# Second slot of a mixture-of-experts kernel: order of loads, index, low terms and register reads

## The chip, the cores and the metric

One Trainium2 chip, one of its cores. The metric is the device time of one execution in microseconds (us), median of three runs. TensorE (matmuls and 128x128 transposes), VectorE, ScalarE and GpSimd work at the same time and are ordered by semaphores alone; SyncE (SP) issues most of the DMAs. GpSimd issues the indirect ones (gather and scatter of rows).

## The reference

```python
def _attn_ref(x, state):                 # x (8, 8, 512, 64), state (8, 8, 32, 64)
    xread = softmax(scale * x @ state.T) @ state
    sread = softmax(scale * state @ x.T) @ x
    return concatenate([xread, sread], axis=2)
# heads are put side by side: 4352 rows of 512
def _moe_ref(x, expert_emb, tau, w1, w2):     # 8 experts, w1 512x1024, w2 1024x512
    logits = normalised(x) @ normalised(expert_emb).T / tau
    e = argmax(logits); gate = softmax(logits)[e]
    return gate * (maximum(x @ w1[e], 0) @ w2[e])
def _moe2_ref(x, w_in, w_out, alpha):         # 512 -> 2048 -> 512
    h = x @ w_in
    return (maximum(h, 0) + alpha * minimum(h, 0)) @ w_out
```

Everything is float32. Each row goes through the two matrices of the one expert with the highest logit.

## The kernel before, in words

Products of float32 are made of three faster ones: each operand is split into a rounded high term and a low term (what rounding left), and `three` (L391 to L395) adds high x high, high x low and low x high. ScalarE mostly makes the high term of a tile, VectorE the low one by a subtraction.

The kernel has three stages. **Attention** runs over the 8 batches (`turn`); its rows go to DRAM (`rows_x`). **Routing and experts** (about 131 to 628 us of the profile): VectorE finds each row's expert and its place, and TensorE turns this into lists of rows (`gather_idx`, `scatter_idx`), 128 rows of one expert to a slot. A slot is: GpSimd gathers the 128 rows into `xg`; TensorE turns them (`transpose_x`, L1621 on), ScalarE and VectorE split them (`xgT_hi`, `xgT_lo`); TensorE makes the hidden rows in two halves (`hidden`, 24 products of 512 columns), VectorE copies each half to `hid`, TensorE turns it, ScalarE and VectorE split it with the relu (`hidT_hi`, `hidT_lo`); TensorE makes the result (`result`, 24 products), ScalarE copies it to `yrow`, GpSimd scatters it. The **last stage** (from about 640 us) is the second network, and the diff does not touch it.

Slots 0 and 1 are written out by hand, because slot 0 starts before the lists are complete: its rows come from a short list of expert 0 (`first_...`), and its work is interleaved with the making of the full lists. VectorE's order there is: `place` (where each row goes in its slot), the small `table` (for each expert its first slot, the number of slots that convert weights, and its end), the two `hidT_lo` of slot 0, the index lists, the low terms of weight chunk 3, the norms and the gate, `xgT_lo` of slot 1. TensorE's is: 8 warm-up products, the rank counts (L1652), `transpose_x(0)`, `hidden`, the index products (L1666), `result` of slot 0, `transpose_x(1)`. GpSimd issues the second gather (L715) as soon as `gather_idx` is complete, with `scatter_idx` and the table to be waited for afterwards (`index_ready` up to `INDEXED`, 8).

The weights of an expert are 4 chunks of 1 MB. SP loads each into one of 4 places of `stage`, ScalarE rounds it to `w_hi`, VectorE subtracts it to `w_lo` (`rest_chunk`, L1001 on). Chunks 0 to 3 (expert 0) pass during attention and slot 0; chunks 4 to 7 (expert 1) are loaded from L499 on, each after the one before has landed, and 6 and 7 only after the second gather has. Chunk 4 needs place 0 (chunk 2 is converted), chunk 5 needs place 1 (chunk 3 is converted).

After that all engines loop over pairs of experts. At the start of each expert ScalarE and VectorE read four numbers of the table into registers (`slots_of`, L386 to L389): start, turns, mid (= start + turns) and end. For expert 0 the start is 1; for each other it is the end of the one before. In the first `turns` slots (at most 2) they also convert the next expert's chunks; an expert with fewer slots has the rest converted at its end. For the first four experts VectorE also makes four sums of blocks of the last stage's weights.

## Time and profile before

| | |
|---|---|
| median of 3 runs | 1375.01 us (1374.06 to 1376.0) |
| the profiled execution's own time | 1372.04 us |
| its span in the profile | 1370.1 us |
| mean granted TensorE clock | 0.992 |
| busy: TensorE, VectorE, ScalarE, GpSimd | 98%, 62%, 31%, 12% of the span |
| experts end at | 321, 371, 383, 440, 503, 565, 615 and 628 us |

The profile is of one execution. Its times are counted from the start of the span; the chain that ended last is 90% TensorE. "Idle before" is what an engine had no work for ahead of an instruction, with the instruction that released it. TensorE's clock is given as a share of 2.4 GHz: 1.00 or, at its lower level, 0.50 (1.2 GHz); a number between them is a mean over a stretch. The end of a matmul is modelled, so the starts are what to go by. A few matmul records are missing.

### The profile page before, as it was taken

How to read it: one execution, taken by the hardware profiler on the slowest of the kernel's cores; microseconds unless marked ns; L12 is line 12 of the kernel's file. 1: busy time of each engine (PE TensorE's matmuls, PEld its weight loads, DVE VectorE, ACT ScalarE, POOL GpSimd, SP SyncE). 2: the span in 40 equal slices, each digit the busy share in tenths (PEclk: the TensorE clock that was granted, in tenths of full speed). 3: DMA queues.
4: the chain of work that ended last, by engine and by line, in shares of the span. 5: the costliest groups of instructions: out<-in, count | busy, mean ns of one | idle time of the engine just before them, and what ended most of it. 6: DMA issues, size and time to landing. Idle time of an engine off the chain costs nothing.

```text
span 1370.1 us, 22457 instructions
## 1 busy us (share of the span) xinstructions
PE 1337.0 (98%) x7820; PEld 1152.7 (84%) x7821; DVE 842.8 (62%) x1106; ACT 424.6 (31%) x611; POOL 166.6 (12%) x228
## 2 busy tenths in 40 slices
PE   8999799999989999998999999999999999999998
PEld 7888578888868888887999999999978888888887
DVE  7898652225474534438667776678966666666652
ACT  6887341114242322325112121113222222222221
POOL 3563121112121121211000000000000000000000
PEclk9999899999999999999999999999999999999999
DMA  8884361114466416234444324343444444444463
GB/s 277 286 280 156 134 221 45 38 46 160 139 225 219 161 44 254 83 124 162 155 141 137 132 109 143 132 144 132 145 126 115 115 115 115 115 115 115 119 118 54
DMA packets 180258, 193.41 MB, mean 141 GB/s; under 512 B 24832, under 2 KB 130304, under 8 KB 179712
## 3 DMA queue, kind: packets, MB, share of 16 engines
q1 hardware_dynamic: 172960, 172.41, 40.4%
q0 software_dynamic: 6112, 19.93, 4.2%
q10 hardware_dynamic: 1152, 0.66, 0.2%
q8 instruction: 17, 0.28, 0.1%
q14 instruction: 17, 0.14, 0.0%
HBM read 125.07 MB, written 67.37 MB: 140 GB/s over the span
## 4 chain that ended last, share of the span: by engine, by line
PE 90%; DVE 6%; DMA 2%; issue 1%; ACT 1%; DVEq 0%; POOL 0%; SPq 0%; ACTq 0%; POOLq 0%
PE ps_p L393 13%; PE ps_p L395 13%; PE ps_p L394 13%; PE ps_y L393 5%; PE ps_y L395 5%; PE ps_y L394 5%; PE ps_h L393 5%; PE ps_h L395 5%; PE ps_h L394 5%; PE ps_o L394 5%; PE ps_o L393 5%; PE ps_o L395 5%; PE ps_hT L1630 2%; PE ps_xT L1624 1%; DVE a L1066 1%; PE ps_sr L1514 1%
## 5 line engine op out<-in xcount | busy, mean ns | idle before, releaser
L393 PE MATMUL ps_p<-b_hi,w_hi 128*128 128x272 f32 x896 | 258.9, 289 | 4.1 <-DVE b_lo L1348 4.1
L395 PE MATMUL ps_p<-b_hi,w_lo 128*128 128x272 f32 x896 | 259.1, 289 | 0.0
L394 PE MATMUL ps_p<-b_lo,w_hi 128*128 128x272 f32 x896 | 259.1, 289 | 0.0
L393 PEld LDWEIGHTS ps_p<-b_hi,w_hi 128*128 128x128 f32 x896 | 169.1, 189 | 5.1 <-DVE b_lo L1348 5.1
L395 PEld LDWEIGHTS ps_p<-b_hi,w_lo 128*128 128x128 f32 x896 | 169.4, 189 | 0.0
L394 PEld LDWEIGHTS ps_p<-b_lo,w_hi 128*128 128x128 f32 x896 | 168.7, 188 | 0.0
L1287 DVE COPY hid<-ps_h 128x512 f32<-128x512 f32 x72 | 49.8, 691 | 171.5 <-PE ps_h L395 166.3
L393 PE MATMUL ps_h<-w_hi,xgT_hi 128*128 128x512 f32 x296 | 121.6, 411 | 3.1 <-DVE xgT_lo L1159 3.1
L393 PE MATMUL ps_y<-w_hi,hidT_hi 128*128 128x512 f32 x296 | 123.3, 417 | 1.2 <-DVE w_lo L1004 0.8
L1415 DVE SCALAR_TENSOR_TENSOR neg<-gt,alpha 128x2048 f32<-128x2048 f32 x33 | 75.6, 2292 | 71.5 <-DMA gt<-acts 71.5
L1426 DVE TENSOR_TENSOR g_lo<-gt,g_hi 128x2048 fp32r<-128x2048 f32 x34 | 77.9, 2292 | 65.5 <-ACT g_hi L964 65.5
L395 PE MATMUL ps_h<-w_hi,xgT_lo 128*128 128x512 f32 x296 | 117.6, 397 | 0.0
L394 PE MATMUL ps_h<-w_lo,xgT_hi 128*128 128x512 f32 x296 | 117.4, 396 | 0.0
L395 PE MATMUL ps_y<-w_hi,hidT_lo 128*128 128x512 f32 x296 | 116.5, 394 | 0.0
L394 PE MATMUL ps_y<-w_lo,hidT_hi 128*128 128x512 f32 x296 | 116.3, 393 | 0.0
L393 PE MATMUL ps_p<-w_hi,g_hi 128*128 128x512 f32 x272 | 107.5, 395 | 1.3 <-issue 1.3
L395 PE MATMUL ps_o<-w_hi,g_lo 128*128 128x512 f32 x272 | 107.4, 395 | 0.0
L394 PE MATMUL ps_o<-w_lo,g_hi 128*128 128x512 f32 x272 | 107.4, 395 | 0.0
L393 PE MATMUL ps_o<-w_hi,g_hi 128*128 128x512 f32 x272 | 107.4, 395 | 0.0
L394 PE MATMUL ps_p<-w_lo,g_hi 128*128 128x512 f32 x272 | 107.4, 395 | 0.0
L395 PE MATMUL ps_p<-w_hi,g_lo 128*128 128x512 f32 x272 | 107.4, 395 | 0.0
L1163 DVE SCALAR_TENSOR_TENSOR hidT_lo<-ps_hT,hidT_hi 128x512 fp32r<-128x512 f32 x74 | 51.1, 691 | 87.9 <-ACT hidT_hi L860 87.9
(258 smaller groups left out, 2345.6 us busy)
## 6 DMA issues: line engine op xcount, KB each, us to landing
acts<-gb SPq DMA_DIRECT2D x128, 272.0 KB, 2.1
stage<-in_moe_w SPq DMA_DIRECT2D x32, 1024.0 KB
gt<-acts SPq DMA_DIRECT2D x32, 1024.0 KB, 6.1
xN_all<-in_xN SPq DMA_DIRECT2D x8, 1024.0 KB, 6.3
rows_x<-xrow SPq DMA_DIRECT2D x32, 256.0 KB, 2.7
out_rows<-orow SPq DMA_DIRECT2D x32, 256.0 KB, 2.0
yz<-rows_y SPq DMA_DIRECT2D x30, 256.0 KB
xs_all<-in_xT SPq DMA_DIRECT2D x7, 1024.0 KB, 6.8
```

The source lines that it names most:

```text
L393: pe.matmul(out, s_hi, m_hi, start=start, stop=False)
L394: pe.matmul(out, s_hi, m_lo, start=False, stop=False)
L395: return pe.matmul(out, s_lo, m_hi, start=False, stop=stop)
L1066: dve.tensor_scalar(a2[par][:, g, :], a2[par][:, g, :], cinv[:, g:g + 1], None, ALU.mult)\
L1163: dve.scalar_tensor_tensor(out=hidT_lo[:, c, :, :], in0=ps_hT[c][:], scalar=0.0, in1=hidT_hi[:, c, :, :].bitcast(F32), op0=ALU.max, op1=AL ...
L1287: dve.tensor_copy(hid[:, c, :], ps_h[c][:]).then_inc(h_copied, 1)
L1415: dve.scalar_tensor_tensor(out=neg[:], in0=gt[k % 2][:], scalar=0.0, in1=alpha[:].unsqueeze(2).to_broadcast([P, KFF, P]), op0=ALU.min, op1 ...
L1426: dve.tensor_tensor(g_lo[k % 2][:], gt[k % 2][:], g_hi[k % 2][:].bitcast(F32), ALU.subtract)\
L1514: mm = pe.matmul(ps_sr[0:NS, h * D:(h + 1) * D], a2T[:, h // GH, cc, (h % GH) * NS:(h % GH + 1) * NS], xN[par][:, cc, h * D:(h + 1) * D], ...
L1624: mm = pe.transpose(ps_xT[:, k, :], xg[:, k * P:(k + 1) * P], ident[:])
L1630: mm = pe.transpose(ps_hT[c][:, k, :], hid[:, c, k * P:(k + 1) * P], ident[:])
```

## The change

It does the following.

- SP holds the load of chunk 5 until the second gather has landed (before: only chunks 6 and 7).
- The low terms of chunks 2 and 3 are made in two halves (`rest_half`). The first half of chunk 2 moves into the last attention turn, that of chunk 3 ahead of the wait for the rank counts; it has a semaphore of its own (`fourth_half_ready`).
- On VectorE the order after `place` is now: `hidT_lo` of slot 0's first half, `gather_idx`, `hidT_lo` of the second half, the table, `scatter_idx`, the second half of chunk 3.
- TensorE turns slot 1's rows after the first 6 of the 12 products of `result(1)`, not after all of them and the wait for the table; it waits for chunk 3's first half before, and for all of it after.
- 6 warm-up products in place of 8.
- `slots_of` reads two numbers (turns and end) and keeps the start in a register from the expert before; mid is their sum.

```diff
@@ -324,6 +324,7 @@
         norm_clamped, norm_root = sem("norm_clamped"), sem("norm_root")
         gate_diff, gate_exp, gate_ready = sem("gate_diff"), sem("gate_exp"), sem("gate_ready")
         first_hot_ready, first_ranked = sem("first_hot_ready"), sem("first_ranked")
+        fourth_half_ready = sem("fourth_half_ready")
         first_placed, first_summed = sem("first_placed"), sem("first_summed")
         onehot_ready, ranks_ready = sem("onehot_ready"), sem("ranks_ready")
         in_slot_ready = sem("in_slot_ready")
@@ -383,10 +384,19 @@
             return nc.s_assert_within(slot, 0, SLOTS - 1,
                                       skip_runtime_bounds_check_because="an expert's first slot and those after it")
 
-        def slots_of(eng, e):
-
-            return [eng.value_load(table[0:1, k, bass.ds(e, 1)], min_val=0, max_val=CT if k == 1 else SLOTS)
-                    for k in range(4)]
+        def first_slot(eng):
+
+            held = eng.alloc_register()
+            eng.reg_mov(held, 1)
+            return held
+
+        def slots_of(eng, e, held):
+
+            turns = eng.value_load(table[0:1, 1, bass.ds(e, 1)], min_val=0, max_val=CT)
+            end = eng.value_load(table[0:1, 3, bass.ds(e, 1)], min_val=0, max_val=SLOTS)
+            start = eng.snap(held, min_val=0, max_val=SLOTS)
+            eng.reg_mov(held, end)
+            return start, turns, eng.snap(start + turns, min_val=0, max_val=SLOTS), end
 
         def three(pe, out, s_hi, s_lo, m_hi, m_lo, start, stop):
 
@@ -495,9 +505,9 @@
                 sp.dma_start(stail[at:at + NS, NS * (b - 1) // P, :], srow[:]).then_inc(tail_loaded, 16)
                 sp.dma_start(rows_x[XT * P + NS * (b - 1) + 1:XT * P + NS * b + 1, :], srow[:]).then_inc(sr_stored, 16)
             store_tokens(B)
-            for i in range(2):
-                load_weights(CH + i, i, expert_chunk(1, i), 3 + i)
+            load_weights(CH, 0, expert_chunk(1, 0), 3)
             sp.wait_ge(gathered, 32)
+            load_weights(CH + 1, 1, expert_chunk(1, 1), 4)
             for i in range(2, CH):
                 load_weights(CH + i, i, expert_chunk(1, i))
             def load_raw(k):
@@ -884,10 +894,11 @@
                 act.wait_ge(x_stored[i], 16 * B)
             act.wait_ge(sr_stored, 16 * B)
             act.sem_inc(yrow_ready, 1)
+            act_slot = first_slot(act)
             with act.Fori(0, E // 2) as pair:
                 for par in range(2):
                     e = 2 * pair + par
-                    start, turns, mid, end = slots_of(act, e)
+                    start, turns, mid, end = slots_of(act, e, act_slot)
                     with upto(act, 0, turns) as i:
                         s = within(start + i)
                         result_before(s)
@@ -1004,6 +1015,13 @@
                 dve.tensor_tensor(w_lo[buf][:, bass.ds(i * CW, CW)],
                                   stage[:, bass.ds(spot, 1), :].rearrange("p a c -> p (a c)"),
                                   w_hi[buf][:, bass.ds(i * CW, CW)].bitcast(F32), ALU.subtract).then_inc(w_lo_ready, 1)
+
+            def rest_half(q, i, spot, half):
+
+                dve.wait_ge(w_hi_ready, q + 1)
+                at = slice(i * CW + half * (CW // 2), i * CW + (half + 1) * (CW // 2))
+                return dve.tensor_tensor(w_lo[0][:, at], stage[:, spot, half * (CW // 2):(half + 1) * (CW // 2)],
+                                         w_hi[0][:, at].bitcast(F32), ALU.subtract)
 
             def rest_scores(b, par, g):
 
@@ -1072,6 +1090,7 @@
                         step(dve.tensor_scalar(lanes_below, iota_p[:].unsqueeze(2).to_broadcast([P, P, 2]), float(-P), None,
                                                ALU.add))
                         dve.tensor_scalar(n2c[:, XT:TE], n2[:, XT:TE], TINY, None, ALU.max).then_inc(norm_clamped, 1)
+                        rest_half(2, 2, 0, 0)
                         copy_srow(b)
                     dve.wait_ge(s1_exp, b + 1)
                     dve.tensor_reduce(rsum[:], heads(a1[par][:]), AX.X, ALU.add).then_inc(s1_sum, 1)
@@ -1126,7 +1145,7 @@
                 step(dve.reciprocal(ninv[:, c], nden[:, c]))
 
 
-            rest_chunk(2, 2, 0, 0)
+            rest_half(2, 2, 0, 1).then_inc(w_lo_ready, 1)
             for k in range(2):
                 dve.wait_ge(tr_copied, 4 * (B - 1) + k + 3)
                 dve.tensor_tensor(a1T_lo[:, k, :].rearrange("p (c t) -> p c t", c=SC), ps_tr[k],
@@ -1195,6 +1214,7 @@
             step(dve.tensor_tensor(lg[:, XT:NT, :], ps_tail, emb_w[:].unsqueeze(1).to_broadcast(to_tail), ALU.mult))
             most(XT - SC, NT)
             choice(XT - SC, NT)
+            rest_half(3, 3, 1, 0).then_inc(fourth_half_ready, 1)
 
             dve.wait_ge(ranks_ready, 1)
             for e in range(E):
@@ -1228,6 +1248,14 @@
                 dve.tensor_tensor(place[:, k, :, :], lanes.unsqueeze(1).to_broadcast(n),
                                   pairs(lo_b[:])[:, k, :].unsqueeze(2).to_broadcast(n), ALU.is_equal)\
                    .then_inc(places_ready, 1)
+            for i in range(SC):
+                dve.wait_ge(x_stored[i], 16 * B)
+            rest_hidden(0, 0)
+
+            dve.wait_ge(index_summed, 1)
+            step(dve.tensor_scalar(idx_h[:], ps_idx[:, 0, :], float(P), None, ALU.mult))
+            dve.tensor_tensor(gather_idx[:], ps_idx[:, 1, :], idx_h[:], ALU.add).then_inc(gather_ready, 1)
+            rest_hidden(0, 1)
             step(dve.tensor_scalar(turns_f[:, 1:E], need[0:1, 1:E], float(CT), None, ALU.min))
             step(dve.tensor_scalar(turns_f[:, 0:1], need[0:1, 0:1], -1.0, float(CT), ALU.add, ALU.min))
             dve.tensor_scalar(table[0:1, 0, 0:1], need[0:1, 0:1], 0.0, 1.0, ALU.mult, ALU.add).then_inc(index_ready, 1)
@@ -1236,20 +1264,12 @@
             dve.tensor_scalar(table[0:1, 2, 0:1], turns_f[:, 0:1], 1.0, None, ALU.add).then_inc(index_ready, 1)
             dve.tensor_tensor(table[0:1, 2, 1:E], first[0:1, 1:E], turns_f[:, 1:E], ALU.add).then_inc(index_ready, 1)
             dve.tensor_copy(table[0:1, 3, :], cum[0:1, :]).then_inc(index_ready, 1)
-            for i in range(SC):
-                dve.wait_ge(x_stored[i], 16 * B)
-            for c in range(2):
-                rest_hidden(0, c)
-
-            dve.wait_ge(index_summed, 1)
-            step(dve.tensor_scalar(idx_h[:], ps_idx[:, 0, :], float(P), None, ALU.mult))
-            dve.tensor_tensor(gather_idx[:], ps_idx[:, 1, :], idx_h[:], ALU.add).then_inc(gather_ready, 1)
             step(dve.scalar_tensor_tensor(out=empty[:], in0=ps_idx[:, 1, :], scalar=0.0, in1=dump[:],
                                           op0=ALU.is_equal, op1=ALU.mult))
             step(dve.scalar_tensor_tensor(out=idx_f[:], in0=ps_idx[:, 1, :], scalar=-1.0, in1=idx_h[:],
                                           op0=ALU.add, op1=ALU.add))
             dve.tensor_tensor(scatter_idx[:], idx_f[:], empty[:], ALU.add).then_inc(index_ready, 2)
-            rest_chunk(3, 3, 1, 0)
+            rest_half(3, 3, 1, 1).then_inc(w_lo_ready, 1)
 
             dve.wait_ge(x_squared, XT)
             dve.wait_ge(tail_squared, NT - XT)
@@ -1293,7 +1313,7 @@
             def experts(pair, sums):
                 for par in range(2):
                     e = 2 * pair + par
-                    start, turns, mid, end = slots_of(dve, e)
+                    start, turns, mid, end = slots_of(dve, e, dve_slot)
                     with upto(dve, 0, turns) as i:
                         slot(within(start + i), CH * (e + 1) + 2 * i, 2 * i, 1 - par)
                         rest_chunk(CH * (e + 1) + 2 * i + 1, 2 * i + 1, 2 * i + 1, 1 - par)
@@ -1312,6 +1332,7 @@
                         dve.wait_ge(s2_made, e + 1)
                         dve.tensor_tensor(sum_w[:, 3], raw_w[:, 1], sum_w[:, 1], ALU.subtract).then_inc(sums_made, 1)
 
+            dve_slot = first_slot(dve)
             with dve.Fori(0, 2) as pair:
                 experts(pair, True)
             with dve.Fori(2, E // 2) as pair:
@@ -1644,7 +1665,7 @@
                                w_second(w_hi[buf], f), w_second(w_lo[buf], f), f == 0, f == KF - 1)
                 return mm
 
-            for _ in range(8):
+            for _ in range(6):
                 pe.matmul(ps_h[0][:], w_hi[0][:, 0:P], w_hi[0][:, 0:DM], start=True, stop=True)
 
             pe.wait_ge(sr_copied, B)
@@ -1665,13 +1686,16 @@
                 pe.wait_ge(places_ready, k // PB + 1)
                 mm = pe.matmul(ps_idx, place[:, k, :, t % 2], marks[:, :, k, :, t % 2], start=(t == 0), stop=(t == NT - 1))
             mm.then_inc(index_summed, 1)
-            for c in range(2):
-                pe.wait_ge(hT_lo_ready, c + 1)
-                pe.wait_ge(w_lo_ready, 3 + c)
-                mm = result(c, range(KF // 2), 0)
-            mm.then_inc(y_ready, 2)
+            pe.wait_ge(hT_lo_ready, 1)
+            pe.wait_ge(w_lo_ready, 3)
+            result(0, range(KF // 2), 0)
+            pe.wait_ge(hT_lo_ready, 2)
+            pe.wait_ge(fourth_half_ready, 1)
+            result(1, range(0, 2), 0)
+            transpose_x(1)
+            pe.wait_ge(w_lo_ready, CH)
+            result(1, range(2, KF // 2), 0).then_inc(y_ready, 2)
             pe.wait_ge(index_ready, INDEXED)
-            transpose_x(1)
             def slot(s, buf, e):
                 pe.wait_ge(xT_lo_ready, s + 1)
                 hidden(0, range(KD), buf).then_inc(h_ready, 1)
```

## Rows read from the trace of the kernel before

**Rows 1.** The page, part 1: busy time of engines, share, instructions.

```profile
PE 1337.0 (98%) x7820; PEld 1152.7 (84%) x7821; DVE 842.8 (62%) x1106; ACT 424.6 (31%) x611; POOL 166.6 (12%) x228
```

**Rows 2.** Timeline, 108 to 140: start, us, engine, line, what, [idle before, releaser].

```profile
123.50 0.68 DVE L1019 COPY srow<-ps_sr 32x512 f32<-32x512 f32 x1 [1.54 <-PE ps_sr L1514]
...
127.08 3.40 DVE L1004 TENSOR_TENSOR w_lo<-stage,w_hi 128x2048 fp32r<-128x2048 f32 x1
...
131.94 0.36 PE L393 MATMUL ps_turn<-stB_hi,a1T_hi 128*128 128x264 f32 x1 [0.94 <-DVE a1T_lo L1132]
```

**Rows 3.** Timeline, 140 to 160; then the chain's two gathers, and all gathers' landing.

```profile
140.02 3.15 PE L1648 MATMUL ps_h<-w_hi 128*128 128x512 f32 x8
...
143.69 0.23 DVE L1201 TENSOR_TENSOR_SCAN counts<-ps_x,offset 128x34 f32<-128x34 f32 x1 [1.29 <-PE ps_x L1653]
...
145.50 0.69 DVE L1159 TENSOR_TENSOR xgT_lo<-ps_xT,xgT_hi 128x512 fp32r<-128x512 f32 x1 [0.27 <-ACT xgT_hi L856]
...
153.37 1.54 PE L1666 MATMUL ps_x<-marks,place 128*128 128x88 bf16 x34
...
153.80 0.15 DVE L1231 TENSOR_SCALAR turns_f<-need 1x7 f32<-1x7 f32 x1
...
154.58 1.27 DVE L1163 SCALAR_TENSOR_TENSOR hidT_lo<-ps_hT,hidT_hi 128x512 fp32r<-128x512 f32 x2
...
155.78 0.18 DVE L1245 TENSOR_SCALAR idx_h<-ps_x 128x44 f32<-128x44 f32 x1
...
156.77 2.29 DVE L1004 TENSOR_TENSOR w_lo<-stage,w_hi 128x2048 fp32r<-128x2048 f32 x1
...
156.98 2.91 POOL L715 DMA_INDIRECT xg<-rows_x,gather_idx  x1 [15.72 <-DVE gather_idx L1246]
...
159.15 11.01 SPq L458 DMA_DIRECT2D stage<-in_moe_w  x3
...
140.20 3.87 DMA xg<-rows_x,gather_idx
...
156.98 7.69 DMA xg<-rows_x,gather_idx
...
DMA to landing us min/median/max: 3.3/3.6/7.7
```

**Rows 4.** Second gather's turn, products; windows: the number after POOL is TensorE's clock.

```profile
164.81 1.09 PE L1624 MATMUL ps_xT<-ident,xg 128*128 128x128 f32 x4 [2.57 <-DMA xg<-rows_x,gather_idx]
...
167.38 0.80 PE L393 MATMUL ps_h<-w_hi,xgT_hi 128*128 128x512 f32 x1 [1.48 <-DVE xgT_lo L1159]
...
173.46 0.23 PE ps_h L395
...
140.00:143.00 3.00, 3.00 (x11) 2.02 (x10) 2.12 (x10) 2.63 (x5) 1.06 (x1) 0.62 0.92 302
143.00:150.00 7.00, 4.97 (x23) 3.57 (x23) 5.58 (x23) 1.18 (x2) 0.00 (x0) 0.92 0.01 4
150.00:162.50 12.50, 10.75 (x76) 8.14 (x74) 10.75 (x29) 3.48 (x6) 3.11 (x2) 1.00 0.15 56
...
164.00:167.40 3.40, 1.11 (x5) 0.59 0.30 115
167.40:170.80 3.40, 3.40 (x8) 0.50 0.72 275
```

**Rows 5.** Timeline: slots 1 and 2, start of expert 3, its clock.

```profile
172.88 0.69 DVE L1287 COPY hid<-ps_h 128x512 f32<-128x512 f32 x1 [3.47 <-PE ps_h L395]
...
189.28 0.66 PE L1624 MATMUL ps_xT<-ident,xg 128*128 128x128 f32 x4 [1.03 <-DMA xg<-rows_x,gather_now]
...
392.58 0.69 DVE L1287 COPY hid<-ps_h 128x512 f32<-128x512 f32 x1 [2.79 <-issue]
...
393.33 1.12 PE L1630 MATMUL ps_hT<-ident,hid 128*128 128x128 f32 x4 [5.39 <-DVE hid L1287]
...
392.70:396.10 3.40, 2.77 (x9) 0.50 0.29 89
```

## The prediction

> **What bounds the kernel now.** I read the page first: TensorE is busy for 1337.0 of 1370.1 us [rows 1], so a change away from TensorE's gaps is worth nothing. Then the waits and the timeline gave me the gaps between 125 and 190 us and near 390 us, the only places that the diff touches. There the reader is to see four of them. TensorE waits 0.94 us for VectorE at 131.94 [rows 2]. It has nothing to do from the end of slot 0's result (about 162.25, 2.57 us before its next start) until the second gather lands at 164.67; then its clock is at the lower level, 1.2 GHz, until 170.8 [rows 3, 4]. It waits 1.03 us for the fourth gather at 189.28, and 5.39 us for a copy by VectorE at 393.33 [rows 5].
>
> **The path to the second slot, first piece: the end of attention.** The low terms of weight chunk 2 take VectorE 3.40 us from 127.08 [rows 2]; the two a1T_lo behind them hold TensorE's token reads back by 0.94. The change does half of it at about 122, in VectorE's idle 1.54 us before the copy at 123.50 [rows 2]: half a chunk is about 1.15 (half of the 2.29 of a whole chunk, rows 3), so it costs nothing; GpSimd has rounded the high terms it needs before that. The half that stays is 1.15, or 2.25 with the 1.1 by which the whole one was stretched beside GpSimd's work. It ends between 128.3 and 129.4. a1T_lo can then start when ScalarE's second copy is there, not behind VectorE, and TensorE is next held by its own read_state, which ends near 131.0 (131.94 less its wait). Gain 0.85 (bounds 0.5 and 0.94). All that follows up to the first gather is one dependency chain and moves along.
>
> **Second piece: up to the places.** The first half of chunk 3 goes into VectorE's 1.29 us wait for the rank counts [rows 3]. It waits for ScalarE's rounding of chunk 3 and takes 1.15, so the scans start about 0.3 later relative to the rest; VectorE then idles 0.27 before xgT_lo at 145.50 [rows 3], which takes that up. Price 0 (at most 0.3, if the gather is not later). The 8 warm-up matmuls, 3.15 us from 140.02, become 6 [rows 3]: the rank products are queued behind them, but these then wait for onehot, and the gather's landing decides. Worth 0; what it may do to the clock is a rival.
>
> **Third piece: index ahead of table.** Before, eight small table operations (153.80 to 154.58), two hidT_lo (1.27 from 154.58, so to 155.8) and only then idx_h stand on the path; the index products ended at 154.91 (153.37 + 1.54) [rows 3]. Now only one hidT_lo (0.64) is ahead, which ends before the products, and idx_h follows the products at about 155.0 in the old time. Gain 0.78. hidT_lo(1) comes 0.4 later in the row of work than the index needs, still before TensorE is through with result(0). The table and scatter_idx come after the gather's start, so their price is nothing; GpSimd, ScalarE and VectorE wait for them (INDEXED) no later than they waited before.
>
> **Fourth piece: the gather itself.** From issue (156.98) to landing it took 7.69; the first one took 3.87 with the same size, and over all 39 the median is 3.6 [rows 3]. The difference of 3.82 has two parts. GpSimd spent 2.91 on it instead of the roughly 1.0 of others, exactly while VectorE's chunk-3 low terms ran (156.77 to 159.06): 1.85. The other 1.97 lies beside the 1 MB load that SP put out at 159.15 [rows 3]. The change takes both away: only half a chunk is left (it starts after hidT_lo, table and scatter, some 1.4 us after GpSimd has started, when descriptors are done), and the load waits for the landing. I take the first gather's 3.87, since it is the same instruction on idle queues: gain 3.82 (bounds 1.85, if loads do not matter or its slowness is its own, and 4.4 by the shortest of 3.3). Queued behind the held load on SP are loads 6 and 7, which already waited for that landing, then the sum blocks and expert 2's. Load 5 is wanted by ScalarE only after the first rounding of the slot, about 5 us after it now goes out; expert 0 has twelve more slots, so the queue has time.
>
> The Trainium skill, "DMA: Bandwidth & Descriptors", section "Queues, rings and completion order", speaks against the second part: an engine takes turns between its queues packet by packet. With its 436 GB/s (section "Anatomy of one DMA") I estimate 0.6 us for these 256 KB alone and 1.2 in turns, so the hold would bring 0.6 and not 1.97, and the total below would be 1.4 smaller. Its fit for one such transfer, 2.0 us plus that 0.6, is 2.6 against the traced 3.87; by it the gain would be 1.3 larger. The rows are used for both.
>
> **Fifth piece: turning the rows within result(1).** In the new time the gather goes out at 155.35 (156.98 - 0.85 - 0.78) and lands at 159.2. TensorE does result(0) and the first 6 products of result(1), 18 in all at 0.23 each [rows 4], from 154.1 to about 158.3, so it waits about 0.9. It turns the rows (0.66 at 2.4 GHz as at 189.28, not the 1.09 of 164.81, rows 4, 5: 0.43), then the last 6 products run beside ScalarE's and VectorE's split. The chain turn, split, product needs 2.57 - 0.43 = 2.14 from start to start (164.81 to 167.38, rows 4). Slot 1 starts at 161.45 instead of 167.38. That is the sum 0.85 + 0.78 + 3.82 + 0.43 = 5.88. Two things are queued behind a wait now: result(1)'s last products behind the gather (a cover of 1.4 us inside 2.14, so free as long as the clock is up), and xgT_lo behind the gate's norms on VectorE, which end near 160.4, 0.3 before it is wanted.
>
> **Sixth: the clock.** TensorE worked 1.11 + 3.40 us in the two stretches at 1.2 GHz [rows 4]; at 2.4 GHz this is half, 2.25, of which 0.43 is counted. So 1.8 if the clock stays up. The stall ahead of it shrinks from 2.57 to 0.9, and the next one (1.48) goes, so I take 1.8 (bounds 0 and 1.8).
>
> **Seventh: register reads.** Four reads keep VectorE 2.79 us before hid at 392.58, so 0.70 each; TensorE waits for this copy 5.39 [rows 5]. Two reads less is 1.4, less about 0.2 for the register moves put in: 1.2 (bounds 1.0 and 1.4, plus up to 1.7 if the low clock there, rows 5, goes too: 0.5 for 6 products and their transposes is lost anyway). At the other expert starts VectorE idles over 3 us waiting for TensorE, and the reads are hidden. At slot 1 they were just hidden (hid at 172.88, rows 5): the gate's last step ended at 169.41 (172.88 less 3.47 idle), 2.0 after the slot's start. Now slot 1's first 12 products end at 164.2 and the six after them at 165.6, while the gate ends at 163.5 (it is chained to the slot's start by xgT_lo) and the reads and waits take 3.47 less 1.4: VectorE can copy hid at 165.5, it is there at 166.1, and TensorE waits 0.5. Price 0.5 (0 to 1.5).
>
> **Slot 2's wait** of 1.03 hangs on GpSimd: scatter, its landing, then the gather. Its input, ScalarE's first yrow, moves by as much as the slot, so I leave it: 0 (-1.0 to +1.0).
>
> **Sum.** 5.9 + 1.8 + 1.2 - 0.5 = 8.4. Against the profiled execution's own time of 1372.04 (span 1370.1, the rest 1.9 around it) that gives 1363.6. The median of the runs is 1375.01, 3.0 above it; I subtract from the median: 1366.6.
>
> **Rivals.**
> A, the gather stays slow (its landing is set by something else than that load, or loads 6 and 7, bunched up behind it, slow the third gather as much). For: gathers beside loads landed in anything from 3.3 to 7.7 [rows 3]. Against: the first one. Then 1.97 and the clock's 1.8 stay away: gain 4.6, 1370.4.
> B, the gain moves into later waits: VectorE's gate chain, the third and the fourth gather, each about a microsecond because slots 1 and 2 now start while three loads are in flight back to back. For: GpSimd's chain already decides slot 2. Against: each has its margin by the numbers above. Gain 6, 1369.
> C, slower: the clock. Six products instead of eight stand before slot 0, and the rows show the clock at 0.62 there and 0.92 and 1.00 in the stretches behind [rows 4]. If it did not rise before slot 1, the 5.6 us of slot 0's hidden products and the transposes double (+6.4 on the gather's path), 18 products of the result add 4.2 less the 1.0 of idle, and slot 1 starts low as before: 1375.0 - 8.4 + 6.4 + 3.2 + 1.8 = 1378. It decides from about 6 us more at the lower level. Against: the rank products and the gather's turn come at once behind, and in the trace TensorE's thin work at 143 to 150 (4.97 of 7 us) did not lower it.
> The Trainium skill, "TensorE: Matmul & The Clock Gate", section "What's actually happening", has the lower level as the default that activity lifts, which is C's rule; the 1.00 behind eight products agrees with it, and no row shows six.
> D, nothing changes that can be measured, since the gaps are refilled: 1374.
>
> **Chances.** Forecast 0.60 (1364.5 to 1368.5 by its own bounds), B 0.18, A 0.13, D 0.05, C 0.04. 0.2% is 2.75 us, about what a measurement of this kernel can tell from no change: faster is the forecast, B and A, 0.91; same 0.06 (D and a mild C); slower 0.03. The range is 1363.2, where the 390 us clock and slot 2's wait go as well, to 1370.6, which takes in A.
>
> **What would show it.** Right: the second gather issued near 155.3 with about 1.0 on GpSimd and landing in under 4.2; load 5 issued behind it; slot 1's first product near 161.5 with clock 1.00; a hid copy near 391 instead of 392.58 (less the shift), with about 1.5 of idle before it. Wrong: the gather over 6 us in spite of the hold; the clock low in slot 0 or still low in slot 1; a new wait of TensorE in slot 1 or 2 for hid or xg of over 1.5; the a1T_lo still behind VectorE; a late weight chunk at an expert's start.

## The result and the profile after

| | before | changed |
|---|---|---|
| median of the runs | 1375.22 us (4 runs) | 1363.3 us (4 runs, 1361.49 to 1367.19) |
| ratio of the medians | | 0.9922 (95%: 0.9908 to 0.9936) |
| profiled execution: own time, span, mean clock | 1372.04, 1370.1, 0.992 | 1367.19, 1365.4, 0.991 |

It is faster by 11.9 us, where 8.4 was forecast: 1363.3 against 1366.6, at the low end of the range. The profiled execution is the slowest of the four. Its page differs from [rows 1] by 2.8 us more busy TensorE:

```profile
PE 1339.8 (98%) x7818; PEld 1155.7 (85%) x7819; DVE 843.3 (62%) x1108; ACT 425.0 (31%) x611; POOL 166.2 (12%) x228
```

TensorE was busy for longer with two products less, in a shorter span: more of it ran at the lower clock. The windows (stretch, TensorE busy, mean granted clock, DMA share, GB/s) show where:

```profile
139.00:142.00 3.00, 3.00 (x12) 0.55 0.98 328
...
148.00:151.00 3.00, 3.00 (x8) 0.50 0.00 0
151.00:154.00 3.00, 3.00 (x10) 0.68 0.00 0
154.00:158.00 4.00, 3.75 (x46) 1.00 0.02 4
```

The clock is at 1.2 GHz from the warm-ups until about 153, over most of slot 0's hidden products, and that is what rival C described. Yet the kernel is faster. To read the steps without this, the same kernel was profiled once more (the first experiment, `after_again`, span 1361.6, mean clock 0.992 like the profile of before). Its timeline, in the columns of [rows 2 to 5]:

```profile
130.66 0.39 PE L403 MATMUL ps_turn<-stB_hi,a1T_hi 128*128 128x264 f32 x1
...
152.44 1.54 PE L1687 MATMUL ps_x<-marks,place 128*128 128x88 bf16 x34
...
155.25 0.96 POOL L725 DMA_INDIRECT xg<-rows_x,gather_idx  x1 [15.22 <-DVE gather_idx L1257]
...
156.41 1.22 DVE L1023 TENSOR_TENSOR w_lo<-stage,w_hi 128x1024 fp32r<-128x1024 f32 x1
...
158.63 10.91 SPq L468 DMA_DIRECT2D stage<-in_moe_w  x3
...
158.66 0.66 PE L1645 MATMUL ps_xT<-ident,xg 128*128 128x128 f32 x4 [0.40 <-DMA xg<-rows_x,gather_idx]
...
161.20 0.49 PE L403 MATMUL ps_h<-w_hi,xgT_hi 128*128 128x512 f32 x1 [0.48 <-DVE xgT_lo L1178]
...
162.47 0.37 DVE L1288 RECIPROCAL gate<-gsume 128x34 f32<-128x34 f32 x1
...
165.05 0.69 DVE L1307 COPY hid<-ps_h 128x512 f32<-128x512 f32 x1 [2.21 <-PE ps_h L405]
...
165.79 0.66 PE L1651 MATMUL ps_hT<-ident,hid 128*128 128x128 f32 x4
...
180.41 0.60 PE L1645 MATMUL ps_xT<-ident,xg 128*128 128x128 f32 x4
...
382.46 0.69 DVE L1307 COPY hid<-ps_h 128x512 f32<-128x512 f32 x1 [1.50 <-issue]
...
383.20 1.11 PE L1651 MATMUL ps_hT<-ident,hid 128*128 128x128 f32 x4 [4.10 <-DVE hid L1307]
```

The reader is to see four things. The a1T_lo no longer holds TensorE at 130.66. The second gather costs GpSimd 0.96 and not 2.91, the half subtraction starts at 156.41, when it is through, and the rows are there 3.4 after its issue, not 7.69. Load 5 goes out at 158.63, with the landing. And at 180.41 and 165.79 there is no wait of TensorE at all. Set against the landmarks of before:

| landmark | before | changed | earlier by | forecast |
|---|---|---|---|---|
| token reads resume [rows 2] | 131.94 | 130.66 | 1.3 | 0.85 |
| second gather issued [rows 3] | 156.98 | 155.25 | 1.7 | 1.6 |
| slot 1's first product [rows 4] | 167.38 | 161.20 | 6.2 | 5.9 |
| rows turned in slot 2 [rows 5] | 189.28 | 180.41 | 8.9 | 7.2 |
| hid turned at expert 3 [rows 5] | 393.33 | 383.20 | 10.1 | 8.4 |
| end of the span | 1370.1 | 1361.6 | 8.5 | 8.4 |

The forecast column is the prediction's terms summed to that point (0.85; with 0.78; 5.88; with 1.8 - 0.5; with 1.2). 1.6 of the gain at expert 3 is lost again at the start of the last stage, where the diff touches nothing. The windows of before and, in the second fence, of the changed kernel there:

```profile
642.00:646.00 4.00, 3.09 (x12) 0.57 1.03 397
646.00:650.00 4.00, 2.75 (x19) 1.00 1.04 388
```

```profile
630.00:634.00 4.00, 1.68 (x7) 0.71 0.80 291
634.00:638.00 4.00, 3.25 (x14) 0.50 1.01 380
638.00:642.00 4.00, 4.00 (x18) 0.51 1.03 388
```

The clock is low for about 3.4 us in the one and some 10 in the other (6.8 in the changed kernel's first profile). So the 8.5 at the end of the span agrees with the 8.4 of the forecast in part by luck: it is a gain of 10.1 less a chance loss of 1.6, and a single profile of this kernel can't be trusted to a microsecond or two.

**How the experiments are read.** Over 106 executions of all 13 kernels, the span falls by 0.90 us (95%: 0.78 to 1.02) for each 0.001 of mean granted clock (one level for each kernel, one slope for all). Besides the median I give "at equal clock": the level of the span at a clock of 0.993, with a 95% bound of 0.4 to 0.8 to either side. The runs come from several chips; the level of the kernel before is the same on three of them within 0.2. It is a rough tool (the clock is printed to 0.001), and it takes away what an edit does to the clock itself; where that is the question, the mean span and clock are given. By it the changed kernel is at 1362.2 (10 executions, mean span 1362.3, clock 0.9929) and the one before at 1370.7 (34 executions, 1372.7, 0.9908): 8.5 at equal clock, 10.4 in the mean.

### The profile page after: what moved, and what is told of

Same layout as the page of the kernel before. It is cut to its first block, busy times and chain, and to the rows that moved or that the text cites. A ratio compares the mean times of both kernels' runs of the same rounds, so it can differ in the third digit from the quotient of the medians.

```text
span 1365.4 us, 22360 instructions
## 1 busy us (share of the span) xinstructions
PE 1339.8 (98%) x7818; PEld 1155.7 (85%) x7819; DVE 843.3 (62%) x1108; ACT 425.0 (31%) x611; POOL 166.2 (12%) x228
## 4 chain that ended last, share of the span: by engine, by line
PE 90%; DVE 6%; issue 1%; DMA 1%; ACT 1%; DVEq 0%; POOL 0%; ACTq 0%; SPq 0%; POOLq 0%
PE ps_p L403 13%; PE ps_p L405 13%; PE ps_p L404 13%; PE ps_h L403 5%; PE ps_h L405 5%; PE ps_h L404 5%; PE ps_y L403 5%; PE ps_o L404 5%; PE ps_o L405 5%; PE ps_y L405 5%; PE ps_o L403 5%; PE ps_y L404 5%; PE ps_hT L1651 2%; PE ps_xT L1645 1%; DVE a L1084 1%; PE ps_sr L1535 1%
```

## The experiments

All ratios below are to the kernel before on the same chip in the same set of runs; each has 5 to 6 executions.

**The changed kernel once more.** No edit.

> The changed kernel again, nothing edited. In its first profile TensorE's clock was at 1.2 GHz for 13.7 us from the end of attention until past slot 0's hidden products (mean clock 0.991, span 1365.4), while two other executions had a mean clock of 0.995 and spans of 1360.2 and 1359.7. If that long stretch is a matter of the moment at which an execution meets the clock's changes, the runs here fall into two groups some 4.5 to 5.5 us apart (about 1361.5 and about 1366.5) that go with their mean clock (0.995 and 0.991). If it is a property of the kernel, the runs are one group within 2 us.

1363.78 us (1362.08 to 1366.92), 0.9926 (0.991 to 0.9943). Its rows stand above. The first profile has the clock low for 13.7 us at slot 0, this one for 6.8, which are over by the time slot 0's hidden products start (145.43): the length differs between executions of one and the same program.

**Rival C: eight warm-ups again.**

```diff
-            for _ in range(6):
+            for _ in range(8):
```

> The changed kernel with 8 warm-up products ahead of the rank counts instead of 6. If the missing two products are what leaves the clock low through slot 0 in some executions, these runs are all in the faster group, near 1361.5, with a mean clock of 0.995, and the median is 0.5 to 2 us lower than that of the kernel with 6. If the number of warm-ups does nothing for it (rival), both kernels show the same mix of groups, and the median differs by less than 1 us. If the products hold the rank counts back, 0.3 to 0.6 us slower in each group.

1364.27 us, 0.9926 (0.9911 to 0.994), 1362.6 at equal clock, mean clock 0.993. Its profile has the low stretch too, after eight warm-ups, for about 10 us:

```profile
138.50:142.00 3.50, 3.38 (x14) 0.72 0.96 307
142.00:145.50 3.50, 1.17 (x5) 0.50 0.00 1
...
149.00:152.50 3.50, 3.50 (x14) 0.81 0.00 0
```

`hold_only` (below), which has eight warm-ups and everything ahead of slot 0 as before, has a low stretch of about 10 us as well: 0.69, 0.50 and 0.53 in the windows 140 to 144, 144 to 148 and 148 to 152. So the two products taken out are not its cause. Ahead of the fall TensorE does the thin products of routing, in both kernels alike; the last three experiments put wide ones among them. The Trainium skill, "TensorE: Matmul & The Clock Gate", section "What's actually happening", says of a kernel's start that the number of products at the lower clock differs between runs of one kernel. The two profiles of the changed kernel show the same in mid-kernel (13.7 against 6.8 us).

**Idle products between the turn and the hidden rows of slot 0.**

```diff
             transpose_x(0)
+            for _ in range(5):
+                pe.matmul(ps_h[0][:], w_hi[0][:, 0:P], w_hi[0][:, 0:DM], start=True, stop=True)
```

> The changed kernel with 5 more idle products put between turning slot 0's rows and its hidden products, where TensorE waits about 1.5 us for the split. If TensorE's idle time before slot 0 is what keeps its clock low there, the long low stretch is gone: every run near 1361.5 with mean clock 0.995. If the clock is low through slot 0 all the same, the filling costs: at 1.2 GHz five products take 2.1 us against 1.5 of wait, so 0.5 us slower in these executions. If filling has no bearing, median as of the changed kernel within 1 us.

1363.97 us, 0.9919 (0.9905 to 0.9934), 1361.9 at equal clock: the same. Filling this gap alone changes nothing that can be measured.

**The load not held.** Rival A and the turn-taking of the Trainium skill ("DMA: Bandwidth & Descriptors", section "Queues, rings and completion order") both speak of it.

```diff
-            load_weights(CH, 0, expert_chunk(1, 0), 3)
+            for i in range(2):
+                load_weights(CH + i, i, expert_chunk(1, i), 3 + i)
             sp.wait_ge(gathered, 32)
-            load_weights(CH + 1, 1, expert_chunk(1, 1), 4)
```

> The changed kernel with the load of chunk 5 no longer held for the second gather. The gather lands in 3.0 us in the changed kernel (issue 159.55, turned at 162.78) against 7.7 before. If it was the load on the DMA engines that made the old gather slow (theory), the load here goes out as chunk 3 is done, about 2.5 us after the gather's issue, and the gather takes 4 to 6 us: 1 to 2.5 us slower than the changed kernel, plus up to 2 more by the clock. Rival: VectorE's chunk-3 subtraction on GpSimd's back and the order of the index made all of the difference, and with those in place the load comes too late to disturb the gather: within 0.7 us of the changed kernel. Then the hold matters only for which transfers slots 2 and 3 meet.

1362.75 us, 0.992 (0.9905 to 0.9935), 1362.6 at equal clock: the hold is worth nothing that can be measured in the changed kernel. The timeline shows what is different:

```profile
155.91 0.95 POOL L725 DMA_INDIRECT xg<-rows_x,gather_idx  x1 [15.22 <-DVE gather_idx L1257]
...
158.38 11.00 SPq L468 DMA_DIRECT2D stage<-in_moe_w  x3
...
159.31 0.66 PE L1645 MATMUL ps_xT<-ident,xg 128*128 128x128 f32 x4 [0.38 <-DMA xg<-rows_x,gather_idx]
```

The load goes out 2.5 after the gather, before its landing, and still the gather lands within 3.4. Before, it went out 2.2 after the gather's issue [rows 3], hardly earlier; but then GpSimd was still writing for another 0.7 (2.91 in all), and here it has been through for 1.5. The load meets a gather that is nearly over. That this is the reason is argued from these rows; no run varied the distance alone.

**The hold alone,** on the kernel before.

```diff
-            for i in range(2):
-                load_weights(CH + i, i, expert_chunk(1, i), 3 + i)
+            load_weights(CH, 0, expert_chunk(1, 0), 3)
             sp.wait_ge(gathered, 32)
+            load_weights(CH + 1, 1, expert_chunk(1, 1), 4)
```

> The kernel before with one edit: the load of chunk 5 is held until the second gather has landed. The order on VectorE is the old one, so chunk 3's subtraction (2.3 us) still begins as GpSimd writes the gather's descriptors. By the prediction's split of the old 7.7 us (1.85 by the subtraction, 1.97 by the load), the gather takes 5.7 us from issue to landing here, GpSimd still 2.9 of it, and the kernel is 2 us faster than before. Rival: the load costs only because the subtraction has pushed the gather's data into it, and alone either is cheap: then too 5.7, since the load is gone. Rival two: the load does nothing, as leaving it in did nothing in the changed kernel: 7 us or more, and no gain.

1369.27 us, 0.9962 (0.9949 to 0.9974): 5.2 off the median of its set, 3.1 at equal clock.

```profile
156.28 1.54 PE L1666 MATMUL ps_x<-marks,place 128*128 128x88 bf16 x34
...
158.87 2.29 DVE L1004 TENSOR_TENSOR w_lo<-stage,w_hi 128x2048 fp32r<-128x2048 f32 x1
...
159.08 2.91 POOL L715 DMA_INDIRECT xg<-rows_x,gather_idx  x1 [17.47 <-DVE gather_idx L1246]
...
164.40 10.62 SPq L458 DMA_DIRECT2D stage<-in_moe_w  x3
...
167.10 0.49 PE L393 MATMUL ps_h<-w_hi,xgT_hi 128*128 128x512 f32 x1 [1.95 <-DVE xgT_lo L1159]
...
172.14 0.69 DVE L1287 COPY hid<-ps_h 128x512 f32<-128x512 f32 x1 [3.47 <-issue]
...
172.88 0.66 PE L1630 MATMUL ps_hT<-ident,hid 128*128 128x128 f32 x4 [1.33 <-DVE hid L1287]
```

This separates the fourth piece. GpSimd still needs 2.91 beside VectorE's whole subtraction, and the gather lands 5.30 after its issue by the chain of waits (7.69 before, 3.37 in the changed kernel). From the end of GpSimd's row to the landing it is 4.8 before (7.69 less 2.91), and 2.4 both here (5.30 less 2.91) and in the changed kernel (3.37 less 0.96). So the load costs 2.4 while the descriptors are written late, and the late writing another 1.9. The two are not additive: an order in which the gather is early against the load makes the hold superfluous. It is also the clearest case of a new wait: with four register reads and a slot that starts sooner, TensorE waits 1.33 for hid. The mean clock is 0.9928 here against 0.9908 before, and slot 1 begins at 1.00 in the profile (windows 164 to 168 and 168 to 172; before 0.58 and 0.57): the clock's gain in slot 1 comes already with the hold alone.

**The turn after all of the result,** and after the wait for the table, as before.

```diff
             result(1, range(0, 2), 0)
-            transpose_x(1)
             pe.wait_ge(w_lo_ready, CH)
...
             pe.wait_ge(index_ready, INDEXED)
+            transpose_x(1)
```

> The changed kernel, with slot 1's rows turned after all of slot 0's result and after the wait for the table, as before. In the changed kernel the gather lands 0.4 us after the first 6 products of result(1); the 6 products that follow (1.4 us) lie beside the split of the rows. Here they lie ahead of the turn: slot 1 starts about 1.1 us later (1.4 less the 0.4 of wait, with the 0.1 by which the last products are late), and the median is 1.1 us higher. Rival: the extra 1.4 us let GpSimd's next gather meet other transfers, and slot 2 waits or does not: 0 or 2 us.

1364.71 us, 0.9926 (0.9911 to 0.9941), 1362.5 at equal clock. From the gather's issue to slot 1's first product its profile has 6.34 (155.38 to 161.72), the changed kernel 5.95 (155.25 to 161.20): the earlier turn is worth 0.4; the 1.1 that I expected was too high. Since the gather lands so early (turn at 158.66, result over at about 159.6 without it), there is not much result left to put beside it.

**Four register reads again.**

```diff
-            turns = eng.value_load(table[0:1, 1, bass.ds(e, 1)], min_val=0, max_val=CT)
-            end = eng.value_load(table[0:1, 3, bass.ds(e, 1)], min_val=0, max_val=SLOTS)
-            start = eng.snap(held, min_val=0, max_val=SLOTS)
-            eng.reg_mov(held, end)
-            return start, turns, eng.snap(start + turns, min_val=0, max_val=SLOTS), end
+            return [eng.value_load(table[0:1, k, bass.ds(e, 1)], min_val=0, max_val=CT if k == 1 else SLOTS)
+                    for k in range(4)]
```

> The changed kernel with all four numbers of the table read at each expert's start, as before. Prediction's step: two reads more, 1.4 us, at expert 3's start where TensorE waits 4.3 us for hid, so that wait becomes 5.4; at slot 1 VectorE's hid is 0.28 late already and becomes 1.4 later: in all 1.1 plus 1.1 to 1.4, 2.2 to 2.5 us slower, and up to 1.7 more where the longer wait brings the lower clock. Rival: the reads are hidden at slot 1, and only expert 3 counts: 1.1 us.

1365.97 us, 0.9939 (0.9924 to 0.9953), 1364.5 at equal clock: 2.3 slower than the changed kernel, as expected. Slot 1 shows half of it, in the same form as `hold_only`:

```profile
168.25 0.69 DVE L1304 COPY hid<-ps_h 128x512 f32<-128x512 f32 x1 [3.48 <-issue]
...
169.00 0.66 PE L1648 MATMUL ps_hT<-ident,hid 128*128 128x128 f32 x4 [1.40 <-DVE hid L1304]
```

"<-issue" where the changed kernel has "<-PE" says little by itself. In `late_turn` the same 2.21 is put down to "<-issue":

```profile
165.97 0.69 DVE L1307 COPY hid<-ps_h 128x512 f32<-128x512 f32 x1 [2.21 <-issue]
```

In the changed kernel too the last of the 12 products that the copy needs had started at 163.87, 1.18 ahead of it. So the 2.21 behind the gate's last step (162.47, 0.37 long) is VectorE's own time in both, and two register reads more make it 3.48. At expert 3 this run has 2.50 of idle before the copy, where the changed kernel's has 1.50.

**Table ahead of the index,** and both hidT_lo, as before.

```diff
-            rest_hidden(0, 0)
-
-            dve.wait_ge(index_summed, 1)
-            step(dve.tensor_scalar(idx_h[:], ps_idx[:, 0, :], float(P), None, ALU.mult))
-            dve.tensor_tensor(gather_idx[:], ps_idx[:, 1, :], idx_h[:], ALU.add).then_inc(gather_ready, 1)
-            rest_hidden(0, 1)
...
             dve.tensor_copy(table[0:1, 3, :], cum[0:1, :]).then_inc(index_ready, 1)
+            for c in range(2):
+                rest_hidden(0, c)
+
+            dve.wait_ge(index_summed, 1)
+            step(dve.tensor_scalar(idx_h[:], ps_idx[:, 0, :], float(P), None, ALU.mult))
+            dve.tensor_tensor(gather_idx[:], ps_idx[:, 1, :], idx_h[:], ALU.add).then_inc(gather_ready, 1)
```

> The changed kernel with VectorE's old order behind the places: the eight table operations, both hidT_lo, then the index. Prediction's step: 0.78 us. The index products end about when the places do, so the gather goes out 0.8 us later and all behind it is 0.8 later; the gather itself takes 3.2 to 3.4 us, as chunk 3's second half still comes after scatter_idx, but now only 0.6 us after the index is complete, so its subtraction runs into GpSimd's descriptors, which then take up to 2 us instead of 0.95: 0.8 by the order alone, 1.8 with this. Rival: in executions with the clock low in slot 0 the index products end so late that VectorE has all of it done before, and the order gives nothing: 0 in these.  In the mean 0.5 to 1.8 us above the changed kernel.

1365.51 us, 0.9942 (0.993 to 0.9955), 1363.2 at equal clock: 1.0 (1.7 in the median) slower.

```profile
154.41 1.54 PE L1687 MATMUL ps_x<-marks,place 128*128 128x88 bf16 x34
...
157.00 1.22 DVE L1023 TENSOR_TENSOR w_lo<-stage,w_hi 128x1024 fp32r<-128x1024 f32 x1
...
157.22 1.84 POOL L725 DMA_INDIRECT xg<-rows_x,gather_idx  x1 [17.42 <-DVE gather_idx L1266]
...
161.32 0.66 PE L1645 MATMUL ps_xT<-ident,xg 128*128 128x128 f32 x4 [1.09 <-DMA xg<-rows_x,gather_idx]
```

With the index last, the half subtraction starts 0.22 before the gather again, and GpSimd is held for as long as it lasts. It ends 0.84 after the subtraction's end here (159.06 and 158.22), 0.83 before (159.89 and 159.06, [rows 3]) and 0.83 in `hold_only`: the 0.95 of an undisturbed gather starts over, as it were, when VectorE is through. The gather takes 4.06 from issue to landing instead of 3.37, which is 0.7 of the 1.0. The index itself is not later in this execution: from the start of the index products to the gather's issue it is 2.81 (154.41 to 157.22), as in the changed kernel (152.44 to 155.25). With the clock low in slot 0 the index products end only at 155.95, and VectorE had the table ready at 153.65; this was the rival of the expectation. The remaining 0.3 is within the bounds. The Trainium skill, "GPSIMD Engine Reference", section "8. Key points", states that GpSimd shares its SBUF interfaces with VectorE and contends with instructions of two SBUF inputs; the trace agrees, and it shows the contention in the time that GpSimd takes to issue a gather.

**Whole chunks** in place of the halves.

```diff
-                        rest_half(2, 2, 0, 0)
...
-            rest_half(2, 2, 0, 1).then_inc(w_lo_ready, 1)
+            rest_chunk(2, 2, 0, 0)
...
-            rest_half(3, 3, 1, 0).then_inc(fourth_half_ready, 1)
...
-            rest_half(3, 3, 1, 1).then_inc(w_lo_ready, 1)
+            rest_chunk(3, 3, 1, 0)
...
-            pe.wait_ge(fourth_half_ready, 1)
+            pe.wait_ge(w_lo_ready, CH)
```

> The changed kernel with the low terms of chunks 2 and 3 whole, in their old places (chunk 3 behind scatter_idx). Chunk 2: a1T_lo is late again, 0.9 us on the path to slot 0. Chunk 3: it ends 1.1 us later, about 4.4 us after the gather's issue, while the gather lands after 3.3; TensorE waits for it with 12 products of result(1) still to do, and turns the rows only after 6 of them: slot 1 starts about 2 us later. GpSimd has written its descriptors by then. In all 2.5 to 3 us above the changed kernel. Rival: the first piece is hidden behind TensorE's read_state (in the changed kernel it no longer waits for a1T_lo, so the whole chunk costs 1.1 at most), and only the second counts: 2 us.

1367.08 us, 0.9955 (0.9942 to 0.9968), 1364.8 at equal clock: 2.6 slower. The 0.96 at the end of attention is back (131.70, waiting for a1T_lo), and the wait of the result for chunk 3, which was 0.83 in the profile of before (159.21), is 1.99:

```profile
131.70 0.36 PE L403 MATMUL ps_turn<-stB_hi,a1T_hi 128*128 128x264 f32 x1 [0.96 <-DVE a1T_lo L1150]
...
158.31 2.28 DVE L1015 TENSOR_TENSOR w_lo<-stage,w_hi 128x2048 fp32r<-128x2048 f32 x1
...
160.74 0.47 PE L403 MATMUL ps_y<-w_hi,hidT_hi 128*128 128x512 f32 x1 [1.99 <-DVE w_lo L1015]
```

With the index first, chunk 3's subtraction is over only at 160.6, and result(1) stands still for 1.99. The split is what makes the order affordable.

**The low stretch moved, then removed.** `thick` puts 6 idle products of 512 columns among routing's thin ones at 135 to 139; `fill9` puts 4 before and 5 after slot 0's turn; `full_fill` does both (its edits are shown; the helpers that make the products are left out).

```diff
+            def thicken(n):
+                for _ in range(n):
+                    pe.matmul(ps_sr[:], w_hi[0][:, 0:P], w_hi[0][:, 0:DM], start=True, stop=True)
...
+            thicken(1)
             tail_scores(0)
...
+            idle_wide(4)
             transpose_x(0)
+            idle_wide(5)
```

> The changed kernel with 6 idle products of 512 columns put among TensorE's thin ones at the end of attention (one ahead of the tail's first logits, two ahead of the first places, one between, two ahead of the tail's last logits). In every trace so far TensorE's clock falls to 1.2 GHz within the few us of tiny products ahead of slot 0, for 3.4 to 13.7 us. If it is this thin work that brings it down, it stays up here: the low stretch before slot 0 is gone from the trace, mean clock 0.996 or more in most executions, and the median is 2 to 3 us below the changed kernel's. If the fall comes from elsewhere, the mix of clocks is the same, and the idle products cost up to 0.5 us.

> The changed kernel with idle products in both of TensorE's waits ahead of slot 0's hidden products: 4 behind the rank counts (it waits for the first gather) and 5 between the turn and the hidden products. With 5 in the second place alone the mean clock was 0.9936 against 0.9929. If idle time after the thin products is what makes the low stretch last over 3.4 us, it is 3.4 us in all executions now: mean clock 0.995, runs between 1361.5 and 1362.5, no slow group, median 1.5 us below the changed kernel. If the stretch's length is set by when the execution meets the clock's changes alone, the mix stays, and at 1.2 GHz the idle products add up to 1 us.

> Both fillings together: 6 idle products among the thin ones at the end of attention and 9 in the two waits ahead of slot 0. With the first alone the low stretch moved to 146 us, behind the two waits, where it lay on slot 0's hidden products. If it takes thin work or idle time to bring the clock down, there is now none between 130 us and slot 1 and the clock stays up: mean clock 0.997, spans under 1360, median 1360 to 1361.5. If the idle products delay the path more than the clock gives back, 1362 to 1364.5 with a high mean clock.

| | median us | ratio (95%) | mean span | mean clock |
|---|---|---|---|---|
| changed, 10 executions | 1363.3; 1363.78 | 0.9922; 0.9926 | 1362.3 | 0.9929 |
| thick | 1364.44 | 0.993 (0.9916 to 0.9944) | 1362.9 | 0.9945 |
| fill9 | 1364.29 | 0.993 (0.9918 to 0.9942) | 1362.4 | 0.9932 |
| full_fill | 1363.16 | 0.992 (0.9907 to 0.9934) | 1360.9 | 0.9962 |

`thick` keeps the clock up over the warm-ups, and it then falls behind 145.5, onto slot 0's products, for about 3.4 us:

```profile
138.50:142.00 3.50, 2.98 (x16) 1.00 0.94 313
142.00:145.50 3.50, 1.05 (x6) 1.00 0.21 77
145.50:149.00 3.50, 2.87 (x7) 0.58 0.00 0
```

The mean clock is higher and the time is not shorter: a low stretch under warm-ups costs little, one under products up to half its length (a product of 512 columns takes 0.43 at the lower clock and 0.23 at the higher, from start to start in slot 1 of the profile before). With both gaps filled there is none before slot 1:

```profile
138.50:142.00 3.50, 2.62 (x18) 1.00 0.84 307
142.00:145.50 3.50, 2.82 (x15) 1.00 0.07 29
...
149.00:152.50 3.50, 3.25 (x19) 1.00 0.00 0
```

That is worth 1.4 in the mean span and 0.1 to 0.6 in the median, which these runs can't tell from nothing; `fill5` (0.9) and `no_hold` (0.7) are below the changed kernel in the mean span as well. At equal clock `full_fill` is at 1363.8, 1.6 above the changed kernel: the idle products take back over half of the 3.0 that the clock gives (0.0033). The expectations of 2 to 3 us for `thick`, of 1.5 for `fill9` and of a median of 1360 to 1361.5 for `full_fill` did not come true, and no version is shown to be better than the changed kernel.

## Why the prediction was right

The direction, the place and slot 1's start (161.20 against 161.45 forecast; 167.38 less the sum of 5.88 would be 161.50) came out. The prediction also named "the clock low in slot 0" as a sign of being wrong, and the first profile shows it: the forecast of the time held in spite of it. Of the 8.4, 1.8 is for the clock and 6.6 for all else. At equal clock the gain is 8.5 (bound about 0.6), 1.9 more than this 6.6. Step by step:

- **End of attention, 0.85:** right. The landmark moved by 1.3, `whole_chunks` puts it back by 1.04 (130.66 to 131.70), and 0.93 has arrived at the index products (153.37 to 152.44).
- **Chunk 3's first half and six warm-ups, 0:** right; the scan still waits 0.34 for the rank counts (1.29 before), so the half chunk fits in, and `warm8` shows no difference.
- **Index first, 0.78:** right for this pair of profiles, and not for every execution. From the start of the index products to the gather's issue it is 3.61 before [rows 3] and 2.81 in the changed kernel. But `hold_only`, with the old order, has 2.80 (156.28 to 159.08), and so has `table_first`: in both the clock is low in slot 0, the index products come late, and the order gives nothing. The step left this condition out.
- **The gather, 3.82 = 1.85 + 1.97:** total about right (4.3 measured), the attribution half wrong. If the hold is made first it brings 2.4 and the rest 1.9; but once VectorE's subtraction stands behind the descriptors the hold adds nothing (`no_hold`). The step wrote "the change takes both away", and treated two ways to the same gain as two gains that add. The sum did not suffer, since both edits are in the change.
- **The turn-taking of the Trainium skill,** by which the hold would bring 0.6 by the prediction's estimate: the trace disagrees where it can be measured, 2.4 in `hold_only`. The fit of its section "Anatomy of one DMA", 2.6 from issue to landing, is below the 3.2 and 3.4 of the two profiles after, which lie between it and the 3.87 that I took.
- **The turn, 0.43:** right, 0.4 by `late_turn`. 
- **Clock in slot 1, 1.8:** right in place; the stretch at 0.50 at 167 to 171 [rows 4] is at 1.00 in both profiles of the changed kernel. It is partly given back elsewhere, in lengths that differ by execution.
- **Register reads, 1.2 and -0.5:** the first right (382.46 against 392.58 is 10.1 earlier, 1.3 more than in slot 2). The second came out as a mechanism and was put too high: TensorE waits 0.28 for hid in one profile and not at all in the other. The copy came at 165.05 where 165.5 was forecast, because the gate's last step ended at 162.84 and not at 163.5. `regs4`, which brings the reads back at both places, is 2.3 slower: 1.3 at slot 1 and 1.0 at expert 3.
- **Slot 2's wait, 0:** wrong; it was worth 1.03, and this is the largest term that was mis-sized. It hung on the scatter of slot 0, which landed 5.9 after GpSimd was through with it. The first fence is GpSimd before, the second the changed kernel, each with SP's four loads of `raw_w`, which make the sum blocks:

```profile
170.26 2.37 SPq L506 DMA_DIRECT2D raw_w<-in_moe_w_in  x4
...
172.73 1.01 POOL L724 DMA_INDIRECT rows_y<-yrow,scatter_now  x1 [4.72 <-ACT yrow L866]
179.65 1.87 POOL L707 COPY scatter_now<-scatter_idx 128x1 uint32 x1 [5.91 <-DMA rows_y<-yrow,scatter_now]
...
183.00 1.00 POOL L703 DMA_INDIRECT xg<-rows_x,gather_now  x1 [0.79 <-ACT yrow L866]
```

```profile
165.04 1.01 POOL L734 DMA_INDIRECT rows_y<-yrow,scatter_now  x1 [3.62 <-ACT yrow L876]
...
169.63 2.49 SPq L516 DMA_DIRECT2D raw_w<-in_moe_w_in  x4
...
169.94 0.18 POOL L717 COPY scatter_now<-scatter_idx 128x1 uint32 x1 [3.88 <-DMA rows_y<-yrow,scatter_now]
...
171.59 3.08 POOL L713 DMA_INDIRECT xg<-rows_x,gather_now  x1 [0.79 <-POOL gather_now L711]
```

Before, it is 10.3 from the scatter's issue to the next gather's; after, 6.5, and the rows come in time even though this gather then holds GpSimd for 3.08 beside a subtraction of VectorE. The wait is gone in both profiles of the changed kernel, in `no_hold`, and in `hold_only`, where the scatter landed 2.74 after GpSimd was through with it. So neither the hold by itself nor the order and the register reads are needed for it; it comes from the transfers' new places. Before, the scatter went out right behind the four loads of `raw_w`; in the 13 other profiles it went out 3.2 to 4.6 ahead of them and landed 2.7 to 3.9 after GpSimd was through. That points at these loads, but no run moved them alone.

- **Profile to median.** In the mean over all executions the gain is 10.4: 8.5 at equal clock, and 1.9 by the clock (0.9908 to 0.9929, at 0.90 us for 0.001). The 1.8 forecast for the clock is thus right in size, though no profile shows that all of it lies in slot 1. The 2.0 by which 10.4 is above the forecast are in the other terms. The landmarks name 1.7 of it at expert 3: slot 2's wait (1.0), the wait for hid (0.5 forecast, 0 here) and slot 1's start (0.3). In this pair of profiles the gain was hidden by the loss at 630 to 646. From 10.4 to 11.9 it is the scatter of two medians of four; the next set has 11.35. That the result is still inside the range, 0.1 above its low end, owes something to this scatter and to slot 2's wait, which the range's low end had counted in.

Rival A (slow gather) is out at 3.4 us, B (later waits) is out by the table of landmarks; the only new wait is the 0.28 for hid. C's mechanism is real: 13.7 us at the lower clock in the profile of the changed kernel, slot 1 then starting at 165.27 instead of 161.20. But eight warm-ups don't prevent it, neither in `warm8` nor in `hold_only`, so it was no price of this change.

**What stays open:** what decides how long a low stretch lasts in an execution; whether `full_fill` is better than the changed kernel; how the 1.9 from the mean clock divides over slot 1, expert 3 and the rest, which one or two profiles of a kernel can't show; and which transfer held slot 0's scatter back.

## What to carry to other kernels

When a gather is slow, read three rows together: how long GpSimd was on it, what VectorE did in that time, and when the next large load went out. Moving the VectorE work behind the gather may make a hold on the load needless, and two edits that aim at one delay are to be priced together, not added. Keep what an edit does at equal clock apart from what it does to the clock, and compare the profiled execution's mean clock with that of the other runs: here 0.001 was 0.9 us. Ask of each gain by order whether it holds at both clock levels; the index's did not.

## What the runs showed of the hardware

- GpSimd's row of one gather is 0.95 us with no such subtraction beside it, 1.84 beside a VectorE subtraction of 1.22, and 2.91 beside one of 2.29; each time it ended 0.83 or 0.84 after the subtraction. VectorE's own half chunk took 2.34 instead of 1.22 beside a GpSimd subtraction (127.96 in the changed kernel's first profile, GpSimd at 127.49 for 1.72).
- A gather of 128 rows lands 3.4 after issue when a 1 MB load starts 2.5 behind it and the descriptors are out, and 7.69 when the load starts 2.2 behind it and they aren't.
- TensorE's clock fell behind routing's thin products in the profiles of both kernels; in those of `thick` and `full_fill`, with 6 wide products among them, it stayed at 1.00 there. In `thick` it fell later, after windows in which TensorE had little to do (1.05 of 3.50 us busy). Under one program the low stretch was 6.8 us in one execution and 13.7 in another.
- Two register reads less on VectorE (with the register moves put in) took 1.3 us out of its idle time at slot 1 (3.47 and 3.48 to 2.21) and about as much at expert 3 (2.49 to 2.79 in the three profiles with four reads, 1.16 to 1.68 in the others), some 0.6 to 0.7 each.
